# Batch 1's queries and keys split into two rounded parts, its scores three products in place of one fp32 product

## The reference

```python
scores = scale * np.matmul(q, k.transpose(0, 1, 3, 2))
scores = scores + bias[None, :, :, :]
scores = np.where(keep, scores, -1000000000.0)
a = np.exp(scores - max);  a = a / (sum(a) + 1e-09)
attn = np.matmul(a, v)
```

## Time and profile before

| | |
|---|---|
| median of 3 runs | 374.98 us (374.26 to 376.41) |
| the profiled execution | 375.65 us |
| its span, first to last instruction | 373.8 us |
| granted TensorE clock, mean | 0.996 |
| TensorE busy | 362.3 us, 97% of the span |
| VectorE, ScalarE, GpSimd busy | 59%, 47%, 21% |

### The profile page before, as it was taken

How to read it: one execution, slowest core, us unless ns; L and a number is a source line. 1 busy time by engine, 2 the same in 40 slices (tenths; PEclk the granted TensorE clock), 3 DMA queues, 4 the chain that set the end, 5 groups by cost and what they waited for, 6 DMA issues and landing times.

```text
span 373.8 us, 6190 instructions
## 1 busy us (share of the span) xinstructions
PE 362.3 (97%) x2266; PEld 323.9 (87%) x2266; DVE 221.4 (59%) x614; ACT 176.3 (47%) x450; POOL 78.2 (21%) x152
## 2 busy tenths in 40 slices
PE   6898999999999999999999999999999999999994
PEld 2566888888788899999989999998899999998883
DVE  5899687777677678779957680213863444440000
ACT  3997575664857469664255650213553111112221
POOL 5868962224332100000030210001410000000000
PEclk9999999999999999999999999999999999999998
DMA  7933333152412304231100000001151000002222
GB/s 234 409 121 115 94 92 118 40 157 73 130 41 59 142 0 161 67 112 56 58 0 1 3 0 0 2 0 44 58 167 58 0 2 0 1 2 86 86 85 89
DMA packets 11797, 27.70 MB, mean 74 GB/s; under 512 B 1520, under 2 KB 3568, under 8 KB 11760
## 3 DMA queue, kind: packets, MB, share of 16 engines
q1 hardware_dynamic: 11328, 26.95, 21.6%
q10 hardware_dynamic: 432, 0.28, 0.3%
HBM read 24.08 MB, written 3.15 MB: 73 GB/s over the span
## 4 chain that ended last, share of the span: by engine, by line
PE 90%; DVE 3%; POOL 3%; DMA 1%; issue 1%; ACT 0%; SPq 0%; DVEq 0%
PE bank L1499 19%; PE bank L1501 19%; PE bank L1500 19%; PE bank L1468 19%; PE bank L1444 5%; PE bank L1401 5%; PE bank L1422 4%; DVE p_sb L1001 1%; POOL p_sb L585 1%; DMA k_sb<-in_k 1%; POOL w_lo L597 1%; DVE pt_sb L1018 1%; POOL bias L572 0%; POOL w_hi L595 0%; DVE denom L1012 0%
## 5 line engine op out<-in xcount | busy, mean ns | idle before, releaser
L1468 PE MATMUL bank<-xT,w_hi 128*128 128x384 f32 x256 | 71.3, 349 | 0.0
L585 POOL TENSOR_SCALAR p_sb<-p_sb,denom 128x256 f32<-128x256 f32 (+1 forms) x96 | 45.8, 492 | 55.3 <-DVE denom L1012 55.2
L1468 PEld LDWEIGHTS bank<-xT,w_hi 128*128 128x128 f32 x256 | 45.6, 188 | 3.5 <-issue 2.5
L680 ACT ACTIVATE p_sb<-p_sb,row_min 128x256 f32<-128x256 f32 (+1 forms) x96 | 46.3, 487 | 2.2 <-DVE row_min L1001 2.2
L1468 PE MATMUL bank<-xT,w_lo 128*128 128x384 f32 x128 | 44.5, 348 | 0.0
L1499 PE MATMUL bank<-g_hi,w_hi 128*128 128x386 f32 (+1 forms) x128 | 43.3, 338 | 0.0
L1501 PE MATMUL bank<-g_hi,w_lo 128*128 128x386 f32 (+1 forms) x128 | 43.2, 337 | 0.0
L1500 PE MATMUL bank<-g_lo,w_hi 128*128 128x386 f32 (+1 forms) x128 | 43.1, 336 | 0.0
L1038 DVE SCALAR_TENSOR_TENSOR c_sb<-h_sb,conv_sb,c_sb 128x382 f32<-128x382 f32 (+1 forms) x64 | 40.6, 634 | 2.3
L688 ACT COPY pt_sb<-bank 128x512 f32<-128x512 f32 (+1 forms) x41 | 22.6, 551 | 37.6 <-PE bank L1422 37.5
L1001 DVE CUSTOM_DVE_ANT_0 p_sb<-bank,bias 128x256 f32<-128x256 f32 (+1 forms) x96 | 33.2, 399 | 8.0 <-PE bank L1401 6.5
(11 more groups left out here) (96 smaller groups left out, 760.1 us busy)
## 6 DMA issues: line engine op xcount, KB each, us to landing
stage<-in_weights SPq DMA_DIRECT2D x17, 512.0 KB, 3.4
v_sb<-in_v SPq DMA_DIRECT2D x8, 390.0 KB, 3.3
k_sb<-in_k SPq DMA_DIRECT2D x8, 384.0 KB, 3.5
out_dram<-out_sb SPq DMA_DIRECT2D x12, 256.0 KB, 2.0
q_sb<-in_q SPq DMA_DIRECT2D x14, 192.0 KB, 3.1
k_sb<-in_k SPq DMA_DIRECT2D x6, 256.0 KB, 4.0
v_sb<-in_v SPq DMA_DIRECT2D x5, 260.0 KB, 2.6
stage_late<-in_weights SPq DMA_DIRECT2D x2, 512.0 KB, 12.6
```

What stands on the lines that cost most here:

```text
L585: nc.gpsimd.tensor_scalar(probs_h, probs_h, denom[:, u % SLOTS, h:h + 1], 1.0, ALU.mult, ALU.mult).then_inc(scaled, 1)
L680: nc.scalar.activation(p_sb[:, u % SLOTS, h, 0:n], p_sb[:, u % SLOTS, h, 0:n], ACT.Exp, bias=row_min[:, u % SLOTS, h:h + 1], scale=-1.0, a ...
L1468: last = nc.tensor.matmul(banks[5 + j % 3][:, 0:C], w, x, start=r == 0, stop=r == F1_GROUP - 1)
```

## The change

For batch 1 alone (triples 8 to 15), ScalarE makes a rounded copy of a triple's queries (`qs[..., 0, :]`, 128x384) and keys (`ks[..., 0, :]`, 128x512, or 128x768 in triples 12 to 15), and GpSimd subtracts it from the original to get the rest (`qs[..., 1, :]`, `ks[..., 1, :]`). ScalarE does it in steps 17, 19, 23, 25, 29, 31, 35 and 37, ahead of that step's `relu_h`; GpSimd in its steps 19, 21, 25, 27, 31, 33, 37 and 39, behind `scale_probs`. The score of one unit and head is then three fp32r products added up in PSUM. TensorE waits on `qk_split` in place of the loads, and SyncE reloads a slot when its split is done, not when its scores are. The new tensors lie in the upper part of batch 1's `h_sb`, so the clearing of its edge columns comes in two parts, the second in VectorE's step 42.

```diff
--- before.py
+++ after.py
@@ -41,6 +41,8 @@
 K0W, K1W = 4 * P, 6 * P
 V0W, V1W = 4 * 2 * DV, 6 * 2 * DV
 SLOTS = 6
+
+SPLIT_FIRST = 2 * HP
 PT_SLOTS = 4
 
 
@@ -173,6 +175,13 @@
         v0_sb = first("v0_sb", [P, HP, V0W])
         assert first.used <= KF * (S + 2) * 4
 
+
+        halves = Packer("h1")
+        halves.used = 2 * (S + 2) * 4 + 48
+        qs = halves("qs", [P, 2, 2, C], F32R)
+        ks = halves("ks", [P, 2, 2, K1W], F32R)
+        assert halves.used <= KF * (S + 2) * 4
+
         att = Packer("c1")
         bias = att("bias", [P, H, TW])
         q_sb = att("q_sb", [P, 2, C])
@@ -264,6 +273,8 @@
         q_rest, k_rest, v_rest = sem("q_rest"), sem("k_rest"), sem("v_rest")
         q_in = [sem(f"q_in{slot}") for slot in range(2)]
         k_in = [sem(f"k_in{slot}") for slot in range(2)]
+        qk_rounded = sem("qk_rounded")
+        qk_split = sem("qk_split")
         val_in = [sem(f"val_in{slot}") for slot in range(2)]
         chunk_in = [sem(f"chunk_in{i}") for i in range(4)]
         stored = [sem(f"stored{i}") for i in range(2)]
@@ -407,6 +418,13 @@
             pair, r = divmod(F1_GROUP * (j + 1) - 1, 2 * F1_STEP)
             return F1_FIRST + 2 * pair + (1 if r < F1_STEP else 2)
 
+        def key_columns(pg):
+            return K0W if pg // HP % 2 == 0 else K1W
+
+
+        def split_step(pg):
+            return TG * pg // 2 * 2 - 7
+
         def values_of(u):
             g, _, hp, tt, t = place(u)
             rows = v0_sb[:, hp, :] if g == 0 else v_sb[:, u // TG % 2, :]
@@ -495,7 +513,9 @@
                 b, c = divmod(g, 2)
                 slot, n = pg % 2, pg - 2
                 pair = b * HP + hp
-                if n >= HP:
+                if n >= SPLIT_FIRST:
+                    sp.wait_ge(qk_split, 2 * (n - SPLIT_FIRST + 1))
+                elif n >= HP:
                     sp.wait_ge(scored, (TG * n + TG - 1) // 2 + 1)
                 sp.dma_start(q_sb[:, slot, :], q[pg]).then_inc(q_in[slot], 16)
                 if c == 0:
@@ -585,6 +605,15 @@
                     nc.gpsimd.tensor_scalar(probs_h, probs_h, denom[:, u % SLOTS, h:h + 1], 1.0, ALU.mult, ALU.mult
                                             ).then_inc(scaled, 1)
 
+            def split_queries(pg):
+                slot, n = pg % 2, key_columns(pg)
+                pool.wait_ge(qk_rounded, 2 * (pg - SPLIT_FIRST) + 1)
+                nc.gpsimd.tensor_tensor(qs[:, slot, 1, :], q_sb[:, slot, :], qs[:, slot, 0, :].bitcast(F32),
+                                        ALU.subtract).then_inc(qk_split, 1)
+                pool.wait_ge(qk_rounded, 2 * (pg - SPLIT_FIRST) + 2)
+                nc.gpsimd.tensor_tensor(ks[:, slot, 1, 0:n], k_sb[:, slot, 0:n], ks[:, slot, 0, 0:n].bitcast(F32),
+                                        ALU.subtract).then_inc(qk_split, 1)
+
 
             def split_piece(i):
                 n, part = divmod(i + PIECES, PIECES)
@@ -611,6 +640,9 @@
                 scale_probs(u)
                 if u in (1, 3, 5):
                     table(5 + u // 2)
+                for pg in range(SPLIT_FIRST, ALL_TRIPLES):
+                    if split_step(pg) + 2 == u:
+                        split_queries(pg)
                 if PIECE_FIRST <= u < PIECE_FIRST + (NW1 - 1) * PIECES:
                     split_piece(u - PIECE_FIRST)
 
@@ -667,6 +699,15 @@
                 hi = w_chunk(n, w2_hi, wi_hi, w3_hi)
                 nc.scalar.copy(hi, staged(chunk)[:, 0:hi.shape[-1]]).then_inc(w_rounded, 1)
 
+            def round_queries(pg):
+                slot, n = pg % 2, key_columns(pg)
+                act.wait_ge(weighed, GU)
+                act.wait_ge(scored, (TG * (pg - 2) + TG - 1) // 2 + 1)
+                act.wait_ge(q_in[slot], 16 * (pg // 2 - 1))
+                nc.scalar.copy(qs[:, slot, 0, :], q_sb[:, slot, :]).then_inc(qk_rounded, 1)
+                act.wait_ge(k_in[slot], 16 * (pg // 2 - 1))
+                nc.scalar.copy(ks[:, slot, 0, 0:n], k_sb[:, slot, 0:n]).then_inc(qk_rounded, 1)
+
             def round_half(c):
                 cols = slice(c * PIECE, (c + 1) * PIECE)
                 if c == 0:
@@ -698,6 +739,8 @@
                 b, c = divmod(kappa, 2)
                 if c == 0 and m == 0:
                     act.wait_ge(padded, b + 1)
+                if b == 1 and c == 0 and m == 2:
+                    act.wait_ge(padded, B + 1)
                 act.wait_ge(h_done, j + 1)
                 nc.scalar.activation(h_sb[b][:, m, 1 + c * C:1 + (c + 1) * C], banks[5 + j % 3][:, 0:C], ACT.Relu
                                      ).then_inc(left_h, 1)
@@ -764,6 +807,9 @@
                     soften(u + 4)
                 if u in (6, 8):
                     round_half(u // 2 - 3)
+                for pg in range(SPLIT_FIRST, ALL_TRIPLES):
+                    if split_step(pg) == u:
+                        round_queries(pg)
                 for j in range(F1_GROUPS - KF):
                     if relu_step(j) == u:
                         relu_h(j)
@@ -1141,8 +1187,11 @@
                     rest_of_half((u - 7) // 2)
                 if u == GU + 2:
                     dve.wait_ge(weighed, GU)
-                    nc.vector.memset(h_sb[1][:, :, 0:S + 2:S + 1], 0.0).then_inc(padded, 1)
+                    nc.vector.memset(h_sb[1][:, 0:2, 0:S + 2:S + 1], 0.0).then_inc(padded, 1)
                     dve.wait_ge(conv_in, 16)
+                if u == relu_step(2 * KF + 2) - 1:
+                    dve.wait_ge(scored, ALL_UNITS // 2)
+                    nc.vector.memset(h_sb[1][:, 2:KF, 0:S + 2:S + 1], 0.0).then_inc(padded, 1)
                 if u == GU:
                     path_tests()
                 if u in tap_steps:
@@ -1389,6 +1438,18 @@
                     if hp == 2 and tt == 0:
                         pe.wait_ge(q_rest, 16)
                         pe.wait_ge(k_rest, 16)
+                elif u // TG >= SPLIT_FIRST:
+                    pg = u // TG
+                    slot = pg % 2
+                    pe.wait_ge(qk_split, 2 * (pg - SPLIT_FIRST + 1))
+                    for part, (i, j) in enumerate(((0, 0), (0, 1), (1, 0))):
+                        for h in range(2):
+                            rows = slice(h * D, (h + 1) * D)
+                            last = nc.tensor.matmul(score_bank(u, h)[:, u % 2 * 2 * P:u % 2 * 2 * P + n],
+                                                    qs[rows, slot, i, tt * P:(tt + 1) * P],
+                                                    ks[rows, slot, j, at_key:at_key + n],
+                                                    start=part == 0, stop=part == 2)
+                    return last
                 else:
                     pg = u // TG
                     slot = pg % 2
```

## The result

The changed kernel takes 374.43 us (median of 22 runs, 373.69 to 376.56); the kernel before, run beside it, 375.41 us. The ratio is 0.9975, with a 95% interval of 0.9965 to 0.9986: 0.94 us faster, by the interval 0.5 to 1.3. The forecast was 0.65 us faster, 0.9983.

The account below looks back on a forecast made before the run. TensorE, busy 97% of the span, was taken as the bound. From 375.65 us profiled, minus 1.05 for score blocks, plus 0.4 for one late split, gives 375.0, or 374.3 on the median's scale; own range 373.7 to 374.9.

Parts of the forecast that it names:

- The bound: Batch 1's score stretch: TensorE is busy without a gap, so a shorter score block shortens the kernel one for one.
- The fp32r price: Score blocks on TensorE: 0.117 us a 256-column pair, 0.11 for 128; full blocks gain 0.151, mixed lose 0.04, together 1.05 gained.
- The late split: GpSimd's first split, triple 8, ends after TensorE wants unit 24's scores: one wait, 0.4 us taken, 0.3 to 0.7.
- The covers: The other seven splits: added work on ScalarE, GpSimd and VectorE fits in slack and costs TensorE nothing.
- margin of 0.24 us on ScalarE: Gap ahead of the even transposes copy, tightest from step 35 to 36: cover 1.58 us, added copies 1.34.
- GpSimd's 2.2 and 2.9 us: GpSimd's split work, 2.2 us for triples 8 to 11 and 2.9 for 12 to 15, hidden between scalings.
- VectorE's cover of 2.8 us: VectorE's bias ahead of the next score block: up to 1.9 us delay at a 768-column split, 2.8 us cover, free.
- The total: Whole kernel: 1.05 us gained on blocks, 0.4 lost to one wait; 374.3 us on the median's scale.
- Loads that do not hide: Rival at the score blocks: loads wait for their row tile's matmul, steps about 0.22 us, +6.4 us, 381.4; chance 0.12.
- Short products at the fp32 price: Rival at mixed blocks: 128-column fp32r pairs take 0.213 us, block 0.99 against 0.64, total +0.6, 375.6; chance 0.17.
- Several late splits: Rival at the later seven splits: ScalarE's margin or VectorE's cover fails, 2 to 4 us added, 376.5 to 378.5; chance 0.11.
- The fast end: Rival at the score blocks: plain pass lengths, full block gains 0.21 us, mixed 0.16, total -1.9, 373.1; chance 0.10.

Follow-up runs that it names:

- e1: Kernel before, with batch 1's scores as three fp32r products on parts of w_in, nothing rounded or subtracted for them; ratio to before 0.9956.
- e4: Changed kernel with the plain fp32 product kept for the four units of 128 keys, behind the same wait for the split; ratio to before 0.9967.
- e2: Changed kernel with its rounding, subtractions and TensorE's wait on them, but the plain fp32 product for the scores; ratio to before 1.0009.
- e3: Changed kernel with GpSimd's last piece of w_in's split moved from behind unit 18's scaling to behind unit 20's; ratio to before 0.9947.
- e6: Changed kernel with only the first of the three score products, rounded queries times rounded keys; ratio to before 0.9884.
- e7: Changed kernel with the three products of head 0 issued before the three of head 1; ratio to before 0.9987.
- e8: Changed kernel with one more copy of the keys on ScalarE at each of the eight roundings; ratio to before 0.9998.
- e5: Changed kernel with GpSimd's last w_in piece two units later and plain fp32 for the four 128-key units, not waiting for the split; 373.21 us, ratio 0.9938.

## Why the prediction was right

**The bound.** Right: e1's 1.3 us on the blocks came out as 1.27 us of stretch.

**The fp32r price.** 0.117 us a pair was taken, and the steps are 0.11 to 0.12; a full block was to be 0.92 and is 0.90 or 0.91. The gain of a full block was put at 0.151 and is 0.165. The mixed block was to be 0.9 and is 0.83 to 0.91, 0.86 in the mean, so its loss is 0.01, not 0.04. Together 1.28 us against 1.05. That the loads, not the matmuls, set the short units' price was argued before; e4 and the starts beside it show it. The mean of the mixed blocks hides two kinds: 0.91 and 0.88 us where the short unit comes first, 0.83 twice where it comes last, while before the change both orders took 0.85 or 0.86. The prediction had no such difference.

**The late split.** The place and the cause were right, e2 and e3 show both. The size was not: 0.76 us against the 0.4 taken and the 0.7 of the upper bound. From the end of the scaling to the end of the keys' subtraction the sum had 2.29 us, and it is 2.62; and 0.12 us pass from there to TensorE's load, which the sum left out. TensorE's own way to that block is 1.98 us, 0.01 more than before: 2.62 + 0.12 - 1.98 = 0.76. The subtractions were put at 0.96 + 1.28 us. Undisturbed they are 1.01 and 1.28 (e3); in this place 1.12 and 1.58. The 0.3 us more of the second come with VectorE's two-input taps beside it: in all six runs where these stand there (the changed kernel, e2, e4, e6, e7, e8) it takes 1.58 or 1.59 us, and in e3 and e5, where they come behind it, 1.28. No run took the taps away with everything else in place, but the order of the records says the same (see the last section). The Trainium skill's rule of a port pair held for a whole operation ("SBUF — State Buffer", section "SBUF: two separate sides") would allow it, and the trace agrees in kind; the size comes from the rows alone.

**The covers.** The margin of 0.24 us on ScalarE was to be the tightest: 0.27 and 0.30 us in the trace, and e8 shows that it is used up right there. GpSimd's 2.2 and 2.9 us and VectorE's delays cost nothing, by e2. But the prediction had these delays on the wrong operations: it counted 1.9 us on the small ones of the earlier trace rows, and they keep 158 ns in the mean between 52 and 118 us; it is the taps that are held. VectorE's cover of 2.8 us is used up first when the blocks are shorter still, by e6.

**The total.** Two terms were off in opposite ways, 0.23 more gain and 0.36 more wait. That they nearly cancel is luck. The stretch has -0.53, the measured ratio -0.94 (0.5 to 1.3), the forecast was -0.65.

**The rivals.** Loads that do not hide: refuted by the steps of 0.12 us, not 0.22. Short products at the fp32 price: a mixed block would be 1.2 us, and none is over 0.91. Several late splits: one only. The fast end: the full block gained 0.165, between the forecast's 0.151 and that rival's 0.21.

## What to carry to other kernels

Three rounded products in place of a plain fp32 one take four passes down to three at best: in two row tiles 256 columns gained 0.16 us in 1.07, and 128 columns lost, as a pair of their stationary loads takes 0.11 us and a pair of their matmuls 0.06, so split the wide ones only. Where side work is added to an engine, look for the first place at which its result is wanted rather than at the mean load: GpSimd is busy for 27% of the changed kernel's span, yet without a pause for the 21 us ahead of the first split. All that the side work cost was at that place, and moving another task by two units gave back more of the stretch than the whole change had gained. Cover holds at the present pace only: with shorter blocks (e6) a quarter of the gain went to waits for work that had been just in time.

## What was not expected of the hardware

A VectorE operation can be held for the whole of a GpSimd operation: the one-input tap of 0.42 us took 1.71 (e6) and, in the changed kernel, up to 1.38, where 0.74 was the longest before. How long it takes hangs on when it starts, and not when it ends. In the changed kernel the keys' subtractions of triples 13 and 15 end at 89.94 and 106.90, and the taps that started at 88.93 and 105.74 end at 90.16 and 107.12, 0.22 us behind each. In the kernel before, the changed one and e2 to e8, every one-input tap of over 0.6 us between 36 and 130 us ends 0.21 or 0.22 us behind the end of a GpSimd operation, and every two-input tap of over 0.9 us, 0.41 or 0.42 us behind. GpSimd is held in turn: a two-input tap that gets through at 50.67 us, at the end of the queries' subtraction, and ends at 51.09 is followed by the keys' subtraction of 1.58 us, 0.30 too long. VectorE's bias and its sum for `xT`, which read one input from PSUM, keep their 0.42 and 0.55 us beside e3's two subtractions.

The Trainium skill, "SBUF — State Buffer", section "SBUF: two separate sides", has a port pair as an exclusive lock that whichever operation starts first keeps for its whole length; it names GpSimd's operations and those of VectorE in a two-port mode or with two SBUF inputs. The constant 0.22 and 0.41 us behind agree with it, and the two-input taps are of the second kind. Whether the one-input tap runs in such a mode no row says.

The order of issue among the two row tiles did not matter. With all three products of head 0 ahead of those of head 1 (e7), the loads still started two at a time, one for each head's tile by their number, 0.11 to 0.12 us apart, and the block kept 0.91 us. Products in turn would have needed nine steps or more, 1.25 us. The rows do not name the head, so it is read from the count and the length of the block. The Trainium skill, "TensorE: Matmul & The Clock Gate", section "Part 3: Packing small matmuls — row/col tiling", has matmuls starting strictly in program order, and loads overlapping running matmuls only in another row group; the first does not fit this run, the second does not fit or the steps of 0.12 us here. The same section also lets a load go ahead into a background weight buffer, which would fit them. The measurements decide.
